# A second fold stored as two runs in PSUM, a weight load tied to another input load, and a new instruction order

## The reference

```
B, H, S, D = 4, 8, 768, 48                       # batches, heads, steps, head width
for t in range(S):                               # attention, per batch and head
    y[t]  = r[t] @ (state + (u*k[t]) outer v[t])
    state = w[t][:, None] * state + k[t] outer v[t]
x  = y as [B, 768, 384]                          # heads side by side
u  = x + real(fft over 384 of (fft over 768 of x))
un = (u - mean) / sqrt(var + 1e-6)               # per row of 384
out = u + max(un @ w_ch1, 0) @ w_ch2             # w_ch1 [384,1536], w_ch2 [1536,384]
```

## Time and profile before

| | us |
|---|---|
| median of three runs | 191.84 (191.71 to 192.07) |
| the profiled execution, its own time | 191.74 |
| its span from first to last instruction | 189.9 |
| PE busy | 176.5 (93% of the span) |
| DVE, ACT, POOL busy | 149.3, 128.5, 109.3 |
| mean granted clock of PE | 0.982 of full speed |

### The profile page before, as it was taken

One profiled execution on the slowest core, in us unless ns is written; L12 is line 12 of the kernel. 1 busy time (PEld: TensorE's weight loads), 2 busy tenths in 40 slices (PEclk: granted clock), 3 DMA queues, 4 the chain that ended last, 5 costly groups with the idle time before them and its releaser, 6 DMA issues.

```text
span 189.9 us, 4765 instructions
## 1 busy us (share of the span) xinstructions
PE 176.5 (93%) x1840; PEld 115.7 (61%) x1840; DVE 149.3 (79%) x346; ACT 128.5 (68%) x307; POOL 109.3 (58%) x133
## 2 busy tenths in 40 slices
PE   6989999808999999999999999989999999999993
PEld 2555768604567676667676765646666766656661
DVE  6598999831699999998999989969897798364133
ACT  3869788309799995979889987694757535336300
POOL 5059863961779961999999296998851154000000
PEclk9999999995899999999999999999999999999999
DMA  6999899999998990596997798996700033600053
GB/s 157 324 311 257 204 230 185 184 215 197 210 202 163 184 191 3 115 215 137 175 211 174 155 233 134 229 197 127 172 31 2 3 124 60 170 23 0 0 200 131
DMA packets 104152, 29.60 MB, mean 156 GB/s; under 512 B 98881, under 2 KB 103618, under 8 KB 104130
## 3 DMA queue, kind: packets, MB, share of 16 engines
q1 hardware_dynamic: 102178, 26.95, 66.8%
q0 software_dynamic: 1952, 2.36, 7.3%
HBM read 24.19 MB, written 4.72 MB: 152 GB/s over the span
## 4 chain that ended last, share of the span: by engine, by line
PE 69%; DMA 15%; SPq 9%; ACT 3%; POOL 2%; DVE 1%; issue 1%; ACTq 0%; DVEq 0%; POOLq 0%
PE bank L1153 24%; PE bank L1135 22%; DMA in_w<-in_w_dram 7%; SPq L520 6%; DMA in_k<-in_k_dram 6%; PE bank L1086 3%; PE bank L852 3%; PE bank L1060 2%; DMA rkt<-rkh 2%; PE bank L910 2%; SPq L514 2%; PE bank L842 1%; PE bank L907 1%; PE bank L786 1%; PE bank L1111 1%; PE bank L836 1%
## 5 line engine op out<-in xcount | busy, mean ns | idle before, releaser
L1135 PE MATMUL bank<-unt,w 128*128 128x384 bf16 x288 | 55.3, 326 | 0.3 <-ACT ht L1142 0.2
L1153 PE MATMUL bank<-w,ht 128*128 128x384 bf16 (+2 forms) x300 | 53.1, 320 | 0.0
L1142 ACT ACTIVATE ht<-bank 128x384 bf16<-128x384 f32 x82 | 37.7, 498 | 16.5 <-PE bank L1135 15.7
L1153 PEld LDWEIGHTS bank<-w,ht 128*128 128x128 bf16 x300 | 27.8, 98 | 15.6
L1135 PEld LDWEIGHTS bank<-unt,w 128*128 128x128 bf16 x288 | 26.3, 98 | 15.7 <-ACT ht L1142 0.8
L865 DVE TENSOR_TENSOR ah<-bank,msk 128x512 bf16<-128x512 f32 x36 | 23.4, 681 | 5.1 <-PE bank L852 4.8
L471 POOL TENSOR_TENSOR rkh<-in_k,e 128x384 bf16<-128x384 f32 x20 | 20.0, 1000 | 9.4 <-ACT e L801 6.9
L1157 DVE SCALAR_TENSOR_TENSOR osb<-bank,rstd,uf 128x384 f32<-128x384 f32 (+2 forms) x25 | 14.9, 595 | 13.0 <-PE bank L1153 10.0
L471 POOL TENSOR_TENSOR rk<-in_r,in_k 128x384 f32<-128x384 f32 x17 | 17.1, 1003 | 7.2 <-DVE rkh L471 5.7
L485 ACT ACTIVATE lb<-in_w 128x384 bf16<-128x384 f32 (+1 forms) x21 | 12.0, 578 | 11.3 <-DMA in_w<-in_w_dram 11.3
L494 ACT ACTIVATE rkt<-bank 128x512 bf16<-128x512 bf16 (+1 forms) x26 | 17.6, 700 | 1.3 <-PE bank L692 0.6
(11 more groups left out here) (155 smaller groups left out, 371.5 us busy)
## 6 DMA issues: line engine op xcount, KB each, us to landing
out_dram<-osb SPq DMA_DIRECT2D x23, 192.0 KB, 2.1
in_w<-in_w_dram SPq DMA_DIRECT2D x18, 192.0 KB, 4.0
in_r<-in_r_dram SPq DMA_DIRECT2D x18, 192.0 KB, 4.1
in_v<-in_v_dram SPq DMA_DIRECT2D x18, 192.0 KB, 4.0
in_k<-in_k_dram SPq DMA_DIRECT2D x18, 192.0 KB, 3.9
w<-in_moe_w_ch_dram POOLq DMA_DIRECT2D x2, 1152.0 KB, 10.9
in_w<-in_w_dram SPq DMA_DIRECT2D x3, 384.0 KB, 4.1
in_k<-in_k_dram SPq DMA_DIRECT2D x3, 384.0 KB, 4.8
```

Of the source, the lines that this page charges most:

```text
L1135: ins = e.matmul(ps(t)[:, 0:384], W1[:, m, j::NJ] if W2C else W1[:, m, 128 * j:128 * j + 128], unt[:, :, m, :], start=(m == 0), stop=(m == ...
L1142: "act": lambda e, j=j, t=t, ht=ht: e.activation(ht[:, j, :], ps(t)[:, 0:384], ACTF.Relu, scale=-1.0)},
L1153: ins = e.matmul(ps(t)[:, 0:hi - lo], ht[:, j, 128 * x:128 * x + 128], W2[:, j, lo:hi], start=(j == 0), stop=(j == NJ - 1))
```

## The change

1. `rows_four` writes the even columns of a block as one run of 97 and the odd ones as a second run, from column 97 on, both with step 1. What reads them, two DVE additions from PSUM and two additions from the copy `Z4`, now takes them alternately from the two runs (`fwd`, `rev`), 192 columns each in place of 193 and 191. `Z4` and the buffer behind it become a few columns longer.
2. W1's issue on POOL waits for `k` of (1,1) in place of `w` of (0,4).
3. `ORDER`, `BANKS` and `AHEAD` are new throughout: other places for nearly all instructions, 65 operations on another engine than before, and three more unused matmuls (NW 22 for 19). The arithmetic is the same.

```diff
-NW = 19
+NW = 22
-W_AFTER = {"W1": (0, 4, "w"), "W2": (1, 0, "r")}
+W_AFTER = {"W1": (1, 1, "k"), "W2": (1, 0, "r")}
...
     "sp": (
-        "46 96 47 51 52 50 97 98 143 398 99 144 145 457 188 369 372 401 427 146 371 370 399 429 400 523 458 456 "
-        "490 430 428 492 491 493 459 525 524 719 748 526 721 722 806 720 749 750 808 777 779 778 807 751 319 840 "
+        "46 96 51 47 52 50 97 98 143 398 99 144 145 427 369 188 372 146 428 401 371 399 456 370 400 490 523 429 "
+        "458 457 492 430 748 525 491 459 524 493 719 526 720 721 722 749 806 750 777 808 807 778 751 779 319 840 "
...
-                    ins = e.matmul(ps(t)[:, 256 * y + x:256 * y + HE:2], src[:, 2 * y + x, a:a + 128], C4[:, y, HK * x:HK * x + n],
+                    ins = e.matmul(ps(t)[:, 256 * y + HK * x:256 * y + HK * x + n], src[:, 2 * y + x, a:a + 128], C4[:, y, HK * x:HK * x + n],
...
+        HH = HE - 1
+
+        def fwd(v):
+            return v[:, 0:2 * HK].rearrange("p (x m) -> p m x", x=2)[:, 0:HH // 2, :]
+
+        def rev(v):
+            return v[:, 1:1 + HH].rearrange("p (x m) -> p m x", x=2)[:, ::-1, :]
...
-        op("dve", v_1(HE), lambda e: e.tensor_tensor(out=uf[:, kb, lo], in0=ps(t)[:, 0:HE], in1=xb[:, kb, lo], op=ALU.add),
+        op("dve", v_1(HE), lambda e: e.tensor_tensor(out=ul, in0=fwd(ps(t)), in1=xl, op=ALU.add),
...
-        op("dve", v_1(HE), lambda e: e.tensor_tensor(out=uf[:, kb, hi], in0=ps(t)[:, HE - 2:0:-1], in1=xb[:, kb, hi], op=ALU.add),
+        op("dve", v_1(HE), lambda e: e.tensor_tensor(out=uh, in0=rev(ps(t)), in1=xh, op=ALU.add),
...
-        vec(HE, tt(uf[:, kb, lo], uf[:, kb, lo], z, fs[0]), r=[("Z4", kb % 2)], w=[("UF", i, kb)])
-        vec(HE, tt(uf[:, kb, hi], uf[:, kb, hi], z[:, HE - 2:0:-1], fs[1]), r=[("Z4", kb % 2)], w=[("UFh", i, kb)])
+        vec(HE, tt(ul, ul, fwd(z), fs[0]), r=[("Z4", kb % 2)], w=[("UF", i, kb)])
+        vec(HE, tt(uh, uh, rev(z), fs[1]), r=[("Z4", kb % 2)], w=[("UFh", i, kb)])
```

More of the change, by code:

```diff
@@ L359, in bass_rwkv6_finch__then__fnet_fourier_mix_kernel @@
     HE = S // 4 + 1
+    HK = HE // 2 + 1
     HQ = S // 8 + 1
@@ L430, in bass_rwkv6_finch__then__fnet_fourier_mix_kernel @@
     K3 = HTF[0][:, 2304:2304 + 6 * HE]
-    K4 = sb("k4", [3 * DM + 8], BF16)
+    K4 = sb("k4", [3 * DM + 12], BF16)
     CS = K2[:, 0:6 * HE].rearrange("p (q x) -> p q x", q=NP)
@@ L437, in bass_rwkv6_finch__then__fnet_fourier_mix_kernel @@
     DTM = K4[:, 0:3 * DM].rearrange("p (j x) -> p j x", j=3)
-    Z4 = [K4[:, 2 * HE + 2 + 2 * HE * x:4 * HE + 2 + 2 * HE * x].bitcast(FP32) for x in range(2)]
+    Z4 = [K4[:, 2 * HE + 2 + 4 * HK * x:2 * HE + 2 + 4 * HK * (x + 1)].bitcast(FP32) for x in range(2)]
     C4 = K4[:, 0:2 * HE].rearrange("p (y x) -> p y x", y=2)
-    HK = HE // 2 + 1
     DTS = ["DTM%d%s" % (j, x) for j in range(3) for x in ("", "r")]
@@ L1019, in rows_four @@
             op("pe", mm(HK, 2), f, r=[(sn, 2 * y), (sn, 2 * y + 1), ("C4", y, 0), ("C4", y, 1)], w=[t])
+        HH = HE - 1
[3 more added lines that the diff above has]
+            return v[:, 1:1 + HH].rearrange("p (x m) -> p m x", x=2)[:, ::-1, :]
         z = Z4[kb % 2]
         old = set(g.rd.get(("UF", i, kb), ())) | set(g.wr.get(("UF", i, kb), ()))
-        lo, hi = slice(0, HE), slice(HE, DM)
-        op("dve", v_1(HE), lambda e: e.tensor_tensor(out=uf[:, kb, lo], in0=ps(t)[:, 0:HE], in1=xb[:, kb, lo], op=ALU.add),
+        ul, uh, xl, xh = [v[:, kb, c].rearrange("p (m x) -> p m x", x=2) for v in (uf, xb) for c in (slice(0, HH), slice(HH, DM))]
+        op("dve", v_1(HE), lambda e: e.tensor_tensor(out=ul, in0=fwd(ps(t)), in1=xl, op=ALU.add),
            r=[t, ("X", i, kb)], w=[("UF", i, kb)])
-        op("dve", v_1(HE), lambda e: e.tensor_tensor(out=uf[:, kb, hi], in0=ps(t)[:, HE - 2:0:-1], in1=xb[:, kb, hi], op=ALU.add),
+        op("dve", v_1(HE), lambda e: e.tensor_tensor(out=uh, in0=rev(ps(t)), in1=xh, op=ALU.add),
            r=[t, ("X", i, kb)], w=[("UFh", i, kb)]).deps.update(old)
-        o = evict(lambda: z, lambda: ps(t)[:, 256:256 + HE], HE, r=[t], w=[("Z4", kb % 2)])
+        o = evict(lambda: z[:, 0:HE], lambda: ps(t)[:, 256:256 + HE], HE, r=[t], w=[("Z4", kb % 2)])
         if b == R2[0]:
```

## The result

The changed kernel took 183.4 us (182.22 to 184.31, four runs) against 191.78 (189.76 to 192.07, four runs) of the kernel before: a ratio of 0.958, 95% interval 0.949 to 0.968. The forecast was 184.2, range 181.8 to 188.4. The profiled execution took 184.16 with a span of 182.4, PE busy 175.8 of it.

A forecast was written before the change was run, and what follows sets the result against it. PE was taken as the bound, its hole never made up. From 191.74 us: minus 7.1 for the hole, minus 1.0 for columns, plus 0.5 for moved work, gives 184.1; 184.2 as median, range 181.8 to 188.4.

The forecast's parts named there:

- The bound and the cause of the hole: PE bounds; its hole before the first MLP matmul comes from W1 delaying `w` of (1,4), landed at 42.6 us.
- PE's line: PE's own work from 37.43 us to the first MLP group: at most 5.8 us at full speed, ending at 43.2.
- The first MLP matmul at 44.7: With the hole's cause gone, it comes at 44.7 us (43.2 to 46.5) instead of 51.82, gaining 7.1 us (5.3 to 8.6).
- the three lines: Paths to the first MLP matmul: PE's work to 43.2 us, ACT's 23 instructions to 42.0–43.9, W1's landing at 42.2–42.6.
- The first 33 us at 0: Start of the kernel: nearly the same batch 0 loads in the same order, so no change, bounds ±0.6 us.
- The columns at 1.0: 24 matmuls writing contiguous columns save 0.040 us each, 1.0 us off PE, bounds 0 and 1.0.
- Moved work at 0.5 lost: Operations moved between engines add some 1.0 us on full DVE from 50 to 130 us; PE loses 0.5 (0 to 1.0).
- The wait of no effect: W1's new wait on POOL for `k` of (1,1) is over when POOL comes: cost 0, gain 0.
- W2 in time: W2's issue on POOL comes earlier along with the operations ahead of it, so W2 lands before its use: cost 0.
- Slow reading: Rival: DVE reads the two runs slowly in batch 3, PE loses 2.6 us, 186.8 us in all; chance 0.08.
- Thin PE: Rival: PE pauses between 37 and 45 us and the clock falls to half again, 188.3 us; chance 0.12.
- W1 catching `k` of (1,2): Rival: that load lands near 42.6 us, holding POOL and PE; first MLP matmul at 54.0, 193.0 us; chance 0.08.

The follow-up runs named there:

- the old wait: The changed kernel with W1's issue waiting for `w` of (0,4) again, as in the kernel before: 182.73 us (181.85 to 182.89), ratio 0.992 to the kernel before.
- second profile: The changed kernel, unchanged, run and profiled again beside the kernel before: 182.97 us median of 12 (182.22 to 184.90); the kernel before 190.69.
- the short execution of before: The kernel before, unchanged, profiled in an execution without the hole: 183.42 us, first MLP matmul at 43.70.
- the long ones: Profiled executions of the kernel before, unchanged, that have the hole: 191.74 us in the first profile, 190.15 in a later one.
- the second try above: The changed kernel with W1's issue one place earlier on POOL, and `k` of (1,2) exchanged with `w` of (1,5) on SP: 183.17 us, median of ten.
- the first try: The changed kernel with W1's issue one place earlier on POOL, ahead of the fold that waits: 182.99 us, median of ten, ratio 1.003.

## Why the prediction was right, and where it was not

- **The bound and the cause of the hole: right.** PE's loss in the hole is never made up (134.75 to 135.09 us from the first MLP matmul to PE's end with the hole, 134.87 without), and W1 on top of `w` of (1,4) is the cause: exchanged, put back, and seen both ways in one kernel. One row was misread: 0.64 in the window from 48 to 49 us means that full clock came back at 48.7, not at 48.3, which makes PE's line 5.6 us in place of 5.8.
- **That the hole is there: only half right.** I read one execution and three equal times and took it for what the kernel does; the 0.2% that I called the limit of a measurement is no more than the spread of those three; the measured interval is 2% wide. The lead of 0.2 us in the earlier trace rows should have told me that it could go either way. Against the executions without the hole the change is worth nothing that can be measured. A forecast of two cases would have been in place: 4% with it, none without. Over all 62 executions of the kernel before and all 16 of the changed one the means are 187.96 and 183.27, a ratio of 0.975; how often the hole comes differs from chip to chip (4 of 4, 3 of 7, 7 of 20 and 19 of 31 at 189.7 or more).
- **The first MLP matmul at 44.7: 46.61 in the profile**, 45.33 with the old wait and 44.82 in its second profile; the gain 5.2 (6.5 and 7.0) against 7.1, in the profile a little outside its own bounds. W1's line ended last in all three: it landed 0.04 to 0.05 us before that matmul, though in the second profile PE came to it only 0.2 us earlier. Two of the three lines were set too early. ACT's began not with the landing (33.1 forecast, 33.97 measured) but at 35.01, when ACT had done its earlier work; its 23 instructions took 10.9 us, 0.47 each, the upper price. W1's began at 35.88 (34.26 and 34.60), not at 32.4 to 32.8: I priced the fold's new wait at 0.4 us, and W1 went out 1.9 to 3.5 us later than before, since the x and the DVE operation that it needs come later in the new order (at 34.35 and 34.65 in the profile).
- **The first 33 us at 0: wrong by up to 1.3 us in the profile**, by the rate at which PE started (last section).
- **The columns at 1.0: 0.7.** I took the pace of the eight matmuls in the slowest row, 0.083; the mean of all 24 was 0.076.
- **Moved work at 0.5 lost: wrong in sign.** Behind the first MLP matmul the changed kernel is 2.5 us shorter, and the columns are 0.7 of that. Another 0.7 are PE's waits, 0.78 us before and 0.07 after, and they lay in the three windows from 115 to 130 that I mentioned and gave 0.11: PE waited some 0.5 us for a transposing DMA of batch 3, in the short execution of before as in the long ones; those of the two long ones are shown. In the changed kernel's first profile no wait of PE stands there, in its second one of 0.21. The remaining 1.0 are matmuls that follow each other faster, 0.3 of it at line 852, and one matmul of line 782 that moved ahead (0.2); why they are faster isn't shown.

```profile
126.06 0.40 PE L852 MATMUL bank<-rkt 48*128 48x128 bf16 x8 [0.52 <-DMA rkt<-rkh]
...
124.46 0.40 PE L852 MATMUL bank<-rkt 48*128 48x128 bf16 x8 [0.51 <-DMA rkt<-rkh]
```

- **The sum** came out at 184.2 against 184.16 because the first MLP matmul was 1.9 us later than forecast and the rest 2.0 shorter. That is luck, not skill.
- **The wait of no effect: right.** **W2 in time: right in the changed kernel's first profile** (landed 65.03, first used 65.79), 0.37 us late in the second. Its issue stands behind 16 operations after W1, not 14.
- **The rivals.** Slow reading: no. Thin PE: no window was empty, and the clock stayed at full in the second profile, which records it from 6.7 us on. W1 catching `k` of (1,2): no, but for another reason than the one I gave; the fold, and not the new wait, held W1, which went out 2.2 to 2.8 us after that load's issue had ended. What W1 does catch first now is `k` of (1,4) or `v` of (1,2), first used at 47.5 us or later and landed by 46.1. That fits all 16 executions of the changed kernel, which lie within 182.2 to 184.9.

## What to carry to other kernels

Where a small urgent load's issue ends within half a microsecond of the beginning of a large load's on another queue, as here, one profile shows one outcome: take more times of the kernel before, look for two groups, and forecast against each. Do not put the large load behind a wait that holds up its engine's other work; put around it small loads that nobody needs for ten microseconds. And when a stall is taken away, date each line that then decides from the moment when its engine is free, not from the landing that used to hold it.

## What the runs showed of the hardware

**The point at which a load is caught.** Over the 14 profiles, W1's issue on POOL takes 0.95 to 0.98 us. Of the loads of 192 KB issued in the 8 us before, those whose issue on SP had ended when W1's began, or up to 0.06 us after that (the short execution of before), landed 3.3 to 5.3 us after their own start. One whose issue ended 0.18 us after took 5.4, one 0.40 after took 4.9. The first one whose issue ended 0.46 us after or later took 9.0 to 12.0, in each of the 14. The end of the issue sorts them, not its start: one load issued 1.0 us ahead of W1 was caught, its issue having lasted 2.3 us, and one issued 0.3 us ahead was not, its issue having lasted 0.7.

**PE's start.** The profile's clock reads 1.00 from the first microsecond, but the matmuls of 384 columns begin at 0.32 us each and turn to 0.16 between 4.4 and 11.0 us, at different times for the same list of PE: in the changed kernel at about 10.2 in the first profile and by 7.0 in the second. The 1.00 up to there is no measurement. In 13 of the 14 traces the record of the clock begins only with a rise to full (at 4.36 us in the profile of before, 6.74 in the second of the changed kernel, 10.96 in the second try above), and a stretch without a record is printed as 1.00. 0.32 is the pace that these matmuls have where half clock is recorded (in the first try, from 11.88 to 12.20). The changed kernel's first trace has no record at all; from 11.25 us on its matmuls of 384 columns are followed 0.16 to 0.18 us later in 657 of 676 cases and by 0.26 at most, which is full clock. The first and last of the slow ones in the first, on PE's timeline (durations with the way through the array):

```profile
5.25 0.48 PE L642 MATMUL bank<-lb,ht 128*128 128x384 bf16 x1 [0.30 <-ACT lb L485]
...
9.53 0.53 PE L643 MATMUL bank<-lb,ht 128*128 128x384 bf16 x1
```

Between that execution and the one with the old wait, at full rate from 5.4, stand 1.3 us at the first MLP matmul (46.61 and 45.33) and nothing behind it (132.61 and 132.59).
